# The first chunk's tap products 120 columns wide, and its tail copied and mixed in two halves

## The reference, cut to what matters

```python
w = np.exp(weight - weight.max(-1, keepdims=True))     # 8 heads x 7 taps
w = w / (w.sum(-1, keepdims=True) + 1e-09)
out = np.einsum('hk,bskhg->bshg', w, x_unf)            # x_unf: the token and the six before it
...
g = x @ w_gate                                         # 192 -> 1536
x = (g / (1 + np.exp(-g)) * (x @ w_val)) @ w_out       # 1536 -> 192
...
h = x @ w_in                                           # 192 -> 2048
x = np.where(h > 0, h, np.exp(np.minimum(h, 0)) - 1) @ w_out2
```

## Time and profile before

| | us |
|---|---|
| median of 3 runs | 1205.31 |
| lowest, highest | 1205.05, 1205.68 |
| the profiled execution, whole | 1204.38 |
| its span | 1202.6 |
| PE busy in the span | 1197.6 |

### The profile page before, as it was taken

The page is one execution under the profiler, slowest core; times in us unless marked ns, Lnnn a source line. Parts: engine busy times, 40 slices in busy tenths (PEclk is TensorE's granted clock), DMA queues, the critical chain, the costliest instruction groups (busy, mean ns, idle before and its releaser), DMA issues.

```text
span 1202.6 us, 31398 instructions
## 1 busy us (share of the span) xinstructions
PE 1197.6 (100%) x11798; PEld 1024.5 (85%) x11798; DVE 775.7 (65%) x1192; ACT 664.6 (55%) x1111; POOL 702.8 (58%) x520
## 2 busy tenths in 40 slices
PE   9999999999999999999999999999999999999999
PEld 7888888888888988889888898888988889888898
DVE  7887565685656756567665666657667475675665
ACT  6557555464554646546465564655546555465565
POOL 5388566474654746547465474654756556465565
PEclk9999999999999999999999999999999999999999
DMA  7412011121111211012110021100212002120110
GB/s 177 114 49 46 11 34 33 32 44 26 24 23 31 44 31 26 17 31 44 31 35 13 26 44 31 35 17 22 44 31 44 9 22 44 31 44 9 31 33 15
DMA packets 103956, 43.38 MB, mean 36 GB/s; under 512 B 75888, under 2 KB 93936, under 8 KB 103920
## 3 DMA queue, kind: packets, MB, share of 16 engines
q1 hardware_dynamic: 103104, 42.29, 15.8%
q10 hardware_dynamic: 816, 0.59, 0.2%
HBM read 16.12 MB, written 6.29 MB: 19 GB/s over the span
## 4 chain that ended last, share of the span: by engine, by line
PE 100%; ACT 0%; DVE 0%; issue 0%
PE up L882 56%; PE down L882 43%; PE down L1088 0%; ACT in_a_hi L637 0%; DVE stage L723 0%; ACT stage L657 0%; DVE halos L808 0%
## 5 line engine op out<-in xcount | busy, mean ns | idle before, releaser
L443 POOL TENSOR_TENSOR hid_lo<-hidden,hid_hi 128x512 fp32r<-128x512 f32 x435 | 606.8, 1406 | 472.8 <-ACT hid_hi L582 306.8
L882 PE MATMUL down<-out_w,hid_hi 64*128 64x384 f32 x2040 | 300.1, 355 | 0.0
L745 DVE TENSOR_TENSOR hidden<-act,up 128x512 f32<-128x512 f32 x191 | 130.8, 685 | 246.3 <-ACT act L565 246.3
L882 PE MATMUL down<-out_w,hid_lo 64*128 64x192 f32 x2040 | 259.9, 251 | 0.0
L785 DVE TENSOR_SCALAR act<-up 128x512 f32<-128x512 f32 x256 | 164.8, 685 | 111.9 <-PE up L882 111.9
L882 PE MATMUL up<-in_b_hi,up_w_hi 64*128 64x512 f32 x1128 | 223.6, 393 | 0.0
L882 PE MATMUL up<-in_b_hi,up_w_lo 64*128 64x512 f32 x1128 | 223.4, 393 | 0.0
L882 PE MATMUL up<-in_b_lo,up_w_hi 64*128 64x512 f32 x1128 | 223.3, 393 | 0.0
L582 ACT ACTIVATE hid_hi<-hidden 128x512 fp32r<-128x512 f32 x192 | 121.5, 633 | 173.8 <-DVE hidden L745 156.6
L616 ACT ACTIVATE hid_hi<-hidden 128x512 fp32r<-128x512 f32 x256 | 157.0, 628 | 97.7 <-DVE hidden L801 80.7
L601 ACT ACTIVATE act<-act 128x512 f32<-128x512 f32 x256 | 156.1, 631 | 92.1 <-DVE act L785 92.1
(11 more groups left out here) (97 smaller groups left out, 1084.0 us busy)
## 6 DMA issues: line engine op xcount, KB each, us to landing
x_raw<-x_dram SPq DMA_DIRECT2D x136, 64.0 KB, 2.2
out_dram<-stage SPq DMA_DIRECT2D x15, 384.0 KB, 2.7
in_b_hi<-in_b_hi SPq DMA_DIRECT2D x32, 128.0 KB, 2.3
in_b_lo<-in_b_lo SPq DMA_DIRECT2D x32, 128.0 KB, 2.3
swapped<-halves SPq DMA_DIRECT2D x32, 128.0 KB, 2.3
in_a_hi<-in_a_hi SPq DMA_DIRECT2D x30, 128.0 KB, 2.3
in_a_lo<-in_a_lo SPq DMA_DIRECT2D x30, 128.0 KB, 2.3
stage<-w_out_dram SPq DMA_DIRECT2D x7, 384.0 KB, 3.8
```

Of the source, the lines that this page charges most:

```text
L443: return pool.tensor_tensor(hid_lo[:, slot, :], hidden[:, s, :], hid_hi[:, slot, :].bitcast(F32), ALU.subtract)
L745: v.tensor_tensor(hidden[:, f % 2, :], act[:, f % 2, :], val_bank(f, n)[:, :], ALU.mult)\
L882: return nc.tensor.matmul(dst, lhsT, rhs, start=start, stop=stop, skip_group_check=True)
```

## The change

The zeroed tile `taps_head` is now 120 columns wide, its first seven hold the taps, and both tap products stream all 120 columns; what is read from the bank is the same seven columns. One memset is added. `WARM_AFTER` falls from 3 to 2. The tail's copy is made in two halves of the tokens, four copies in place of two, and PE mixes the first half of the tokens (four products of 256 columns) after the first two copies, the second half after the others. DVE waits for `zeroed` before it writes `taps_head`, and no longer before it reads the bank.

```diff
-    WARM_BEFORE, WARM_AFTER = 6, 3
+    WARM_BEFORE, WARM_AFTER = 6, 2
+    WIDE = 120
...
-        taps_head = sb("taps_head", [HEADS, TAPS])
+        taps_head = sb("taps_head", [HEADS, WIDE])
...
-        ZEROED = 6
+        ZEROED = 7
...
-            for rows, ahead in ((TOP, 0), (LOW, 1)):
-                nc.scalar.activation(paired[rows, HALO - ahead:HALO - ahead + T], X_TAIL[rows, :], ACT.Copy)\
-                    .then_inc(paired_done, 1)
+            for t0, t1 in ((0, T // 2), (T // 2, T)):
+                for rows, ahead in ((TOP, 0), (LOW, 1)):
+                    f0, f1 = t0 and t0 + ahead, min(t1 + ahead, T)
+                    nc.scalar.activation(paired[rows, HALO - ahead + f0:HALO - ahead + f1], X_TAIL[rows, f0:f1],
+                                         ACT.Copy).then_inc(paired_done, 1)
...
             v.memset(tap_pairs[:, :], 0.0).then_inc(zeroed, 1)
+            v.memset(taps_head[:, :], 0.0).then_inc(zeroed, 1)
...
-            tap(v.tensor_scalar(taps_head[:, :], taps_exp[:, :], taps_inv[:, 0:1], None, ALU.mult))
+            v.wait_ge(zeroed, ZEROED)
+            tap(v.tensor_scalar(taps_head[:, 0:TAPS], taps_exp[:, :], taps_inv[:, 0:1], None, ALU.mult))
             v.wait_ge(taps_ready, 1)
-            v.wait_ge(zeroed, ZEROED)
-            by_channel = TAPS_PS[:, 0:2 * TAPS].rearrange("p (a k) -> p a k", a=2)
+            by_channel = TAPS_PS[:, 0:2 * WIDE].rearrange("p (a k) -> p a k", a=2)[:, :, 0:TAPS]
...
-                last = mm(TAPS_PS[:, part * TAPS:(part + 1) * TAPS], head_of[:, part, :], taps_head[:, :],
+                last = mm(TAPS_PS[:, part * WIDE:(part + 1) * WIDE], head_of[:, part, :], taps_head[:, :],
                           True, True)
...
-            pe.wait_ge(paired_done, 2)
-            for k in range(PAIRS):
-                pe.wait_ge(diag_done, k + 1)
-                last = mm(MIX0[:, :], diag[:, k, :], paired[:, 2 * k:2 * k + T], k == 0, k == PAIRS - 1)
+            for half in range(2):
+                pe.wait_ge(paired_done, 2 * half + 2)
+                t0, t1 = half * T // 2, (half + 1) * T // 2
+                for k in range(PAIRS):
+                    if half == 0:
+                        pe.wait_ge(diag_done, k + 1)
+                    last = mm(MIX0[:, t0:t1], diag[:, k, :], paired[:, 2 * k + t0:2 * k + t1], k == 0, k == PAIRS - 1)
             last.then_inc(mix0_ready, 1)
```

## The result

| | us |
|---|---|
| before, median of 5 runs | 1205.31 (1205.05 to 1205.97) |
| after, median of 5 runs | 1192.35 (1191.89 to 1193.75) |
| ratio | 0.9896, 95% interval 0.9885 to 0.9907 |
| span of the profiled execution, before and after | 1202.6, 1190.5 |

What follows compares the result with a forecast made beforehand. PE was taken to bound the kernel, the change touching only the first 12.86 us. Head gains of 0.43 to 1.3 us, middle 0.85, gave 1203.5 or 1204.5 depending on scatter; 1204.0 was taken, range 1203.2 to 1205.3.

Steps and rivals of the forecast that it cites:

- What bounds the kernel: Whole span: PE is busy 1197.6 of 1202.6 us, so only work before the first projection at 12.86 us can gain.
- As long as PE never waits later: Behind the head: an earlier first projection is passed on one to one, since PE never waits after 12.86 us.
- The change lies wholly in these 12.86 us.: Head before the first projection: the change touches only this part, 1.1% of the time.
- The clock: PE's head: matmul steps of 0.214 and 0.43 us show the clock rising at about 8.6 us, during the mixing.
- The 0.93 us between the profiled execution and the median: Scatter between executions: clock rises between 9.9 and 11.2 us would explain it, and the change might remove it.
- Wide products: Tap products in the head: streaming 120 columns fills a 1.1 us stretch with next to no columns, costing 0.15 us.
- case A: Rival, chance 0.62: the clock rises before the mixing; gain 0.43 to 1.3 us, time 1204.0.
- Fewer warm records: Warm products before the mixing: two fewer records save 0.43 us of PE before a wait, nothing on the chain.
- rival D: Chance 0.04: with four warm records the clock stays low through the mixing, 3.0 us slower, 1207.4.
- Split copies and mixing: Tail in the head: first two copies end 0.42 us sooner; sixteen mixing records take the same 3.44 us, loads hidden.
- Rival B: Chance 0.24: the clock rises no sooner, only the split is left, gaining 0.15 to 0.4 us; 1205.1.
- The sum of the head: Head: gain 0.43 us with the clock up at the mixing, 1.3 if up at about 5 us; middle 0.85.

Runs made afterwards that it cites:

- e1: Kernel before with only `taps_head` allocated 120 columns wide, seven used, so all tiles behind it lie 448 bytes higher; 1193.57 us, ratio 0.9907.
- e2: Changed kernel with the wide `taps_head` allocated last and a 7-column tile in its old place, so other tiles lie as before; 1204.54 us, ratio 0.9994.
- e14: Kernel before with the weights moved 128 bytes higher, `stage` and all data 256 higher; 1182.80 us, ratio 0.9812.
- e12: Kernel before with an unused tile of 224 bytes in front of `x_raw`; 1208.06 us, ratio 1.0023.
- e18: Kernel before with the wide tap products alone, the 120-column tile allocated last so no other tile moves; 1204.81 us, ratio 0.9995.
- e6: Kernel before with an unused tile of 64 bytes in front of `x_raw`; 1206.23 us, ratio 1.0011.
- e13: Changed kernel with 192 unused bytes in front of `x_raw`, taking its data to the weights' place within 256 bytes; 1182.96 us, ratio 0.9822.
- e3: Kernel before with `WARM_AFTER` 2 in place of 3, one warm product taken out; 1207.26 us, ratio 1.0020.
- e17: Kernel before with split copies and mixing and `WARM_AFTER` 2, but the narrow tap products; 1205.73 us, ratio 0.9999.
- e4: Kernel before with the tail copied and mixed in two halves, nothing else; 1204.65 us, ratio 0.9998.
- e16: Kernel before with 128 unused bytes in front of `x_raw` and 128 more in front of `act`; 1195.61 us, ratio 0.9916.
- e8: Kernel before with an unused tile of 448 bytes in front of `hid_hi`; 1204.45 us, ratio 0.9997.
- e15: Kernel before with 128 unused bytes in front of `hid_hi`, moving `hid_hi`, `hid_lo` and what lies behind; 1201.79 us, ratio 0.9969.
- e7: Kernel before with an unused tile of 256 bytes in front of `x_raw`; 1204.95 us, ratio 1.0002.
- e10: Kernel before with an unused tile of 128 bytes in front of `x_raw`; 1182.47 us, ratio 0.9809.
- e5: Kernel before with an unused 448-byte tile in front of the weights, so weights and data move together; 1205.07 us, ratio 0.9999.

## Why the prediction was wrong

**What bounds the kernel.** Right: PE all along, and what happens to PE's work is passed on one to one. The 12 us came out of PE's busy time. "As long as PE never waits later" holds in the profile of before, and not in all executions: the two waits near 117 and 121 us stand in nine of the twenty.

**"The change lies wholly in these 12.86 us."** This is the step that failed. The diff has a line outside the head's instructions, the allocation of `taps_head`, and the prediction priced only its memset. It moves every tile behind it by 448 bytes relative to the weights. e1 shows 11.8 us from that line alone, e2 shows that without it the rest of the diff is worth 0.9 us by the medians, in an interval that holds zero, and e14 that the distance to the weights is what does it. None of the rivals had this; none of the rows was read for how far the 232 ns of a pair stand above what PE can do, though 3831 such pairs are 889 us of the span. In the best place of those tried a pair takes 227 ns. The 5 ns more before are 20 us (19.6 in the traces of before and e14), the products that stream `out2_w` add 2.6, and no view names any of it as a wait.

**The clock.** The steps of 0.214 and 0.43 us were read rightly. The rise at 8.6 us rests on taking 0.43 for the first mixing step at the upper level; e12, e18 and e6, at the upper level from the start, have 0.50 there. So 0.10 us were too many, not 0.17, and the rise was at about 8.5. The 0.93 us between the profiled execution and the median were put down to a later rise. That is half of it: the rise moves the first projection by up to 2.3 us between executions, and the two waits behind the head add 1.3 us in some, which no change in the head can remove.

**Wide products.** The clock rise before the mixing was forecast as a consequence of the wide products (0.62). In the profile after it was up at 5 us. With the same head, e2 and e13 have it rise during the mixing; e18 has it up at 8.50, when the mixing starts, and e12 and e6 had it up at 5 us without the wide products. So case A is not shown; the chip's own scatter is larger than what was forecast. The last record's cost, taken as 0.15: the tap copies start at 5.29 in e2 against 5.09, 0.20, at the upper bound of 0.19.

**Fewer warm records.** "By themselves they cost and gain nothing on the chain": wrong. e3 is 1.9 us slower (1.0010 to 1.0030), and its profile has the mixing at the lower clock up to the seventh of eight records. The mechanism stood in rival D and was given 0.04 for the change as a whole. With the split (e17) the loss does not show in the median, with split and wide products (e2) neither. Whether the split or the wide products make up for it, or the scatter hides it, stays open.

**Split copies and mixing.** The copies were 0.42 us sooner, as forecast: with two warm products e17 starts the mixing at 7.89 in place of 8.31. In e4 the third warm product holds PE until 7.97, which is what taking it out was for. At the upper level throughout, sixteen records took 3.69 us (after) and eight 3.67 (e12), so the loads stay hidden, as taken. Rival B's 0.15 to 0.4 us are below what the runs resolve (0.9998, 0.9989 to 1.0008).

**The sum of the head.** 1.3 us to the median were forecast, 0.9 measured in e2 with an interval that holds zero. e2 lies in the range, 1203.2 to 1205.3, but that does not bear out case A: in its profile the clock rose during the mixing and the projection started no sooner. The range was one for the head alone, and the head is a small part of what the change did.

**What stays open.** Why operands of PE at equal places within 256 bytes go best, why a distance of 64 is good and 32 and 96 are the worst, and what of a product's history counts (in e16 it is gone after five pairs). The runs show the effect, its period and that weights and data both take part, not the mechanism; that no other engine takes part is argued from the traces. Other distances between the weights of the two blocks, or between `in` and `hid`, were not tried beyond e8, e15 and e16.

## What to carry to other kernels

An allocation that changes size is a change to every tile behind it: look up the layout before and after, and when a diff moves it, run the shift alone first. In a kernel that TensorE bounds, compare the step from one matmul to the next with the smallest that any layout gives; a few ns on each are seen in no wait and were worth 1.9% here, for 128 unused bytes. When executions of one kernel scatter by as much as a change is meant to give, split the profiled span at the end of the part that was changed: here the part behind the head came out at 1189.7 us in before, e3, e4 and e7, whatever the head did. And a warm product that nothing reads can be what brings the clock up in time (1.9 us in e3): take it out only with a measurement of its own.

## What the runs showed of the hardware

- TensorE's steps depend on where weights and data lie to one another within 256 bytes: 227 ns for a pair of 64-row, 512-column records at equal places (e10, e14), 229 at a distance of 64 (after, e1) and 232 at 128 (before), with the products unchanged. Shifts of data and weights together, and of the data by 256, change nothing (0.9999, 1.0002).
- The Trainium skill, in "TensorE: Matmul & The Clock Gate", part 2, says that loading the next tile's weights does not steal read bandwidth from the running matmul, because TensorE has two read ports. Here the time of a matmul stream does depend on the distance of the two operands (227 ns a pair in e10 and e14, 232 in before and e5), so the two reads seem not to be without effect on each other, or on what follows them; that is argued from the distance, and no run here shows the ports.
- The effect reaches past one product: in e15 five pairs took 1.16 us behind a projection and 1.13 behind their like, and in e16 the first five steps of a projection are 228 to 236 ns and the others 226 or 227.
- One DVE instruction (subtraction of 128x768) took 1.1 to 1.3 us in eleven profiled executions and 3.5 to 3.8 in nine, and cost 1.3 us at the end.
- The moment at which TensorE's clock rises scattered between executions with the same head: transposes at 4.75 us were at the upper level in e12 (0.11 us apart), in the kernel before the mixing at 8.31 still began at the lower one (transposes 0.21 apart).
